# A block end's last sums: rounding the upper channels ahead of the quotient, and summing them between two steps of a numerator

## The chip, the cores and the metric

One core of one Trainium2 chip. The metric is the device time of one execution in microseconds (us), median of several runs; one more execution is profiled.

## What is computed

A causal convolution over the sequence (7 taps per head, softmaxed weights), then two dense layers of 192 -> 2048 -> 192 over 8192 tokens, each with a gate on the hidden value:

```python
x = attn_out.reshape(B * S, D)                  # B*S = 8192, D = 192
h = x @ w_in                                    # first layer, w_in 192 x 2048
x = (h * np.clip(h + 3.0, 0.0, 6.0) / 6.0) @ w_out
h = x @ w_in2                                   # second layer
P = a[0] + a[1]*h + a[2]*h**2 + a[3]*h**3       # numerator
Q = 1.0 + abs(b[0])*abs(h) + abs(b[1])*h**2     # denominator
out = (P / (Q + 1e-06)) @ w_out2
```

## The kernel before

Tokens are worked in 16 blocks of 512 (`BLK`), the hidden dimension in 16 tiles of 128 (`NF`), so there are 256 tiles per layer. The 192 channels are split into 128 lower ones ("a") and 64 upper ones ("b"). Each fp32 value is split into a rounded high part (fp32r) and the rest, a low part, and the products are made of several fp32r passes: in_product (L315) has five matmuls of 512 columns per tile, out_product (L327, 328, 329 into `ya_acc`, L332, 333 into `yb_acc`) five more. The two halves (partitions 0 to 63 and 64 to 127) of `yb_acc` are both sums for the same 64 upper channels, and must be added at the end of a block.

The two layers run interleaved. `run` walks a course of steps; step p works tile p of layer 1 and tile s = p - 20 of layer 2, and in each step every engine issues, in the order of its own list in a plan (`START`, `BEGIN`, `RAMP`, `MIDDLE`, `TURN`, `END`), what is due. `MIDDLE` holds from p = 30 to p = 257; from 258 `TURN` or `END`. In a list, ("num1", 1) is the tile s - 1 of layer 2; ("x2b_hi", SUM1, 0) is a step once per block k, issued in the first step with p - SUM1 - 0 >= 16 k, SUM1 being 18. No engine ever leaves its order; whoever waits holds up what stands behind it.

TensorE in a step of `MIDDLE`: in1(p), in2(s), out1(p-2), out2(s-4), 20 matmuls. The layer-1 hidden values have one PSUM bank only (`kept`), so in1(p+1) waits for gate1(p), which reads it (L402). in2 has three banks.

ScalarE per step: rsq2 (L456), relu1 (L395), rec2 (L468, writes the square of rsq, a first guess of 1/Q, over the h bank, and so waits for num1, the last reader of h), sq2 (L435), abs2 (L429), lin2 (L423), g1hi and g2hi (L507: round the gated values of layers 1 and 2; g2hi(s-2) waits for out2(s-4), the last reader of its buffer).

VectorE per step: num2 (L441), num1 (L446), the second and third steps of the numerator's Horner scheme; g_neg (L486, finishes the quotient), gate1 (L402), newton (L472), g_first (L479); in some steps one to three convolution taps (L599, L612) and cs_b_lo (L513). The taps of the upper channels are worked for two blocks at a time, all ahead of blocks of even number.

GpSimd per step: den_sum (L452), g1lo (L416), g2lo (L501), the low parts.

Once per block, in the step whose out1(p-2) is the first tile of the next block (p = 18 + 16 k), the sums of layer 1 leave PSUM: y1a_out (ScalarE, L521), x2a_hi (ScalarE, L507), x2a_lo (GpSimd, L515) for the lower channels; x2b_hi (ScalarE, L507: rounds `yb_acc[0][0:64]` into `xb_hl[1]`; the profile's y0b_acc and x1b_hl), x2b_res (VectorE, L542: what the rounding left, into partitions 64 to 127 of `x2b_rest`) and x2b_lo (VectorE, L547: adds the other half of `yb_acc`) for the upper ones. In that same step the first out1 of the new block may only start on `ya_acc` after y1a_out, and on `yb_acc` (its fourth matmul, L332) after x2b_lo. Both x2b_hi and y1a_out need the last out1 of the block, which TensorE ran one step earlier.

Of the kernel before, what the change touches and what calls it, by code (L numbers as in the profile page):

```python
# [34 lines left out]
SUM1, SUM2 = 16 + OUT1, 20  # L35
AHEAD, PAIR_AHEAD = -16, -32
# [32 lines left out]
MIDDLE = {  # L69
    "sync": [("load_a", AHEAD, 0), ("load_b", PAIR_AHEAD, 0, 0), ("store_y", SUM2, 1)],  # L70
    "tensor": [("in1", 0), ("in2", 0), ("out1", 2), ("out2", 4)],
    "scalar": [("y2b_move", SUM2, 0), ("y2a_out", SUM2, 0), ("x2b_hi", SUM1, 0), ("cs_b_hi", AHEAD, 13, 0),
             ("conv_a_first", AHEAD, -1), ("y1a_out", SUM1, 0), ("rsq2", 1), ("relu1", 0), ("x2a_hi", SUM1, 0),
             ("rec2", 1), ("conv_b_first", PAIR_AHEAD, 11, 0), ("sq2", 0), ("abs2", 0),
             ("cs_b_hi", AHEAD, 5, 1), ("lin2", 0), ("cs_a_hi", AHEAD, 10), ("g1hi", 0), ("g2hi", 2)],
    "vector": [("num2", 1), ("num1", 1), ("cs_b_lo", AHEAD, 15, 0), ("x2b_res", SUM1, 0),
             ("x2b_lo", SUM1, 0), ("y2b_sum", SUM2, 0), ("g_neg", 2), ("gate1", 0), ("newton", 1),
             ("cs_b_lo", AHEAD, 10, 1), ("conv_a", AHEAD, (1, 4, 5, 6, 7, 8)),
             ("conv_b_head", PAIR_AHEAD, (11, 13, 14), 0), ("conv_b_tail", AHEAD, (10, 11, 12), 0),
             ("g_first", 1)],  # L80
# [874 lines left out]
```

## Time and profile before

| | |
|---|---|
| median of 3 runs | 1211.4 us (1211.37 to 1211.76) |
| profiled execution | 1210.91 us, its span 1209.1 us |
| busy: TensorE / weight loads | 98% / 79% |
| busy: VectorE / ScalarE / GpSimd | 96% / 97% / 89% |
| granted TensorE clock, mean | 0.999 |

The span runs from the first to the last instruction. A matmul in the records lasts 0.39 us, but the next starts 0.23 us after it: they overlap, so a busy share of 98% does not say that the array streams without holes; the holes are seen in start times. Weight loads overlap the matmul before them. The granted clock is at its higher level, 2.4 GHz, throughout.

### The profile page before, as it was taken

What the parts mean: (1) busy time and instruction counts of PE and PEld (TensorE: products, weight loads), DVE (VectorE), ACT (ScalarE), POOL (GpSimd) and SP (SyncE); (2) the same over time, 40 slices, a digit from 0 to 9 for tenths busy, and PEclk for the clock granted to TensorE, in tenths of its full rate; (3) what the DMA queues carried; (4) which work ended last, traced back from release to release, by engine and by line L of the source; (5) the groups of instructions that cost most, each with busy time, mean ns of one, the idle gap of its engine ahead of it and who ended that gap; (6) DMA issues with size and microseconds to landing.
All of it is one profiled execution on the core that took longest, in us unless ns stands there. A gap on an engine that the chain in (4) does not pass through costs nothing.

```text
span 1209.1 us, 18307 instructions
## 1 busy us (share of the span) xinstructions
PE 1179.0 (98%) x5136; PEld 961.1 (79%) x5136; DVE 1158.8 (96%) x1786; ACT 1171.2 (97%) x2233; POOL 1070.8 (89%) x832
## 2 busy tenths in 40 slices
PE   6999999999999999999999999999999999999976
PEld 5778788888888888888888888888888888888754
DVE  7899999999999999999999999999999999999898
ACT  7899999999999999999999999999999999999997
POOL 5879989899998999989898998989989899998876
PEclk9999999999999999999999999999999999999999
DMA  4400000000000000010000000000000000000000
GB/s 147 150 1 10 1 23 1 23 10 23 1 1 26 6 23 1 1 32 1 23 1 21 11 1 23 1 23 10 1 23 1 23 1 14 1 1 14 1 14 14
DMA packets 10021, 21.17 MB, mean 18 GB/s; under 512 B 1600, under 2 KB 1856, under 8 KB 9920
## 3 DMA queue, kind: packets, MB, share of 16 engines
q1 hardware_dynamic: 9632, 20.00, 5.7%
q8 instruction: 40, 0.66, 0.2%
q14 instruction: 61, 0.50, 0.1%
q10 hardware_dynamic: 288, 0.01, 0.0%
HBM read 13.72 MB, written 6.29 MB: 17 GB/s over the span
## 4 chain that ended last, share of the span: by engine, by line
PE 78%; ACT 9%; DVE 6%; issue 5%; POOL 2%; DMA 0%; ACTq 0%; POOLq 0%; DVEq 0%
PE h L315 39%; PE y0b_acc L332 4%; PE y0b_acc L333 4%; PE y0a_acc L327 4%; PE y0a_acc L329 4%; PE y0a_acc L328 4%; PE y1a_acc L327 4%; PE y1a_acc L328 4%; PE y1a_acc L329 4%; PE y1b_acc L332 4%; PE y1b_acc L333 4%; ACT g_hi L507 2%; ACT num L423 1%; ACT sqr L435 1%; DVE num L441 1%
## 5 line engine op out<-in xcount | busy, mean ns | idle before, releaser
L452 POOL TENSOR_TENSOR den<-den,sqr 128x512 f32<-128x512 f32 x246 | 355.5, 1445 | 96.8 <-ACT den L429 92.6
L501 POOL TENSOR_TENSOR g_lo<-g,g_hi 128x512 fp32r<-128x512 f32 x255 | 331.0, 1298 | 2.5 <-ACT g_hi L507 2.5
L416 POOL TENSOR_TENSOR g_lo<-r,g_hi 128x512 fp32r<-128x512 f32 x235 | 308.7, 1314 | 4.5 <-ACT g_hi L507 2.8
L446 DVE SCALAR_TENSOR_TENSOR num<-num,coef,h 128x512 f32<-128x512 f32 x246 | 183.9, 748 | 8.4
L479 DVE SCALAR_TENSOR_TENSOR h<-num,coef,h 128x512 f32<-128x512 f32 x238 | 178.1, 748 | 0.2
L441 DVE TENSOR_TENSOR num<-num,h 128x512 f32<-128x512 f32 x246 | 167.9, 683 | 10.3 <-ACT num L423 4.4
L507 ACT ACTIVATE g_hi<-g 128x512 fp32r<-128x512 f32 x256 | 167.0, 652 | 10.2 <-DVE g L486 2.4
L423 ACT ACTIVATE num<-h,coef 128x512 f32<-128x512 f32 x246 | 175.0, 711 | 0.2
L402 DVE SCALAR_TENSOR_TENSOR r<-r,h 128x512 f32<-128x512 f32 x235 | 160.8, 684 | 9.2 <-ACT r L395 8.4
L456 ACT ACTIVATE rsq<-den 128x512 f32<-128x512 f32 x246 | 157.5, 640 | 7.8 <-POOL den L452 5.2
L486 DVE SCALAR_TENSOR_TENSOR g<-den,h 128x512 f32<-128x512 f32 x238 | 161.8, 680 | 0.7
L472 DVE SCALAR_TENSOR_TENSOR den<-den,h 128x512 f32<-128x512 f32 x238 | 161.8, 680 | 0.7 <-ACT h L468 0.4
L507 ACT ACTIVATE g_hi<-r 128x512 fp32r<-128x512 f32 x235 | 155.3, 661 | 0.0
L395 ACT ACTIVATE r<-h 128x512 f32<-128x512 f32 x256 | 153.8, 601 | 1.4 <-PE h L315 1.4
L435 ACT ACTIVATE sqr<-h 128x512 f32<-128x512 f32 x246 | 149.5, 608 | 1.4
L429 ACT ACTIVATE den<-h 128x512 f32<-128x512 f32 x246 | 150.3, 611 | 0.0
L468 ACT ACTIVATE h<-rsq 128x512 f32<-128x512 f32 x240 | 146.6, 611 | 0.8 <-DVE conv_b L446 0.2
L327 PE MATMUL y1a_acc<-g_hi,wout 128*128 128x512 f32 x255 | 100.8, 395 | 10.3 <-POOL g_lo L501 7.8
L315 PE MATMUL h<-x1a_hi,win_hi 128*128 128x512 f32 x256 | 100.1, 391 | 2.7 <-DVE g L486 2.4
L332 PE MATMUL y0b_acc<-g_hi,wout 128*128 128x512 f32 x256 | 101.0, 395 | 1.7 <-DVE x1b_hl L547 1.2
L327 PE MATMUL y0a_acc<-g_hi,wout 128*128 128x512 f32 x256 | 100.1, 391 | 2.4 <-DVE g_lo L416 1.4
L315 PE MATMUL h<-x0a_hi,win_hi 128*128 128x512 f32 x256 | 100.8, 394 | 0.7 <-DVE y1b_acc L402 0.4
(143 smaller groups left out, 2970.9 us busy)
## 6 DMA issues: line engine op xcount, KB each, us to landing
stage_w<-w_pack SPq DMA_DIRECT2D x16, 448.0 KB, 3.4
raw_a<-x_a SPq DMA_DIRECT2D x16, 259.0 KB, 3.2
out<-y_a SPq DMA_DIRECT2D x16, 256.0 KB, 2.0
out<-y_b SPq DMA_DIRECT2D x16, 128.0 KB, 2.3
raw_b<-x_b SPq DMA_DIRECT2D x14, 129.5 KB, 2.7
raw_b<-x_b SPq DMA_DIRECT2D x4, 65.5 KB, 4.7
tap_ab<-taps ACTq DMA_DIRECT2D x1, 7.0 KB, 3.3
coef<-coefs ACTq DMA_DIRECT2D x1, 3.0 KB, 4.2
```

What stands on the lines that cost most here:

```text
L315: mm = eng.matmul(psum, w, x[:, :], start=(i == 0), stop=(i == len(passes) - 1))
L327: eng.matmul(ya_acc[l][:, :], a_hi, g_hi[:, :], start=first, stop=False)
L332: eng.matmul(yb_acc[l][:, :], b_hl, g_hi[:, :], start=first, stop=False)
L416: eng.tensor_tensor(g1_lo[t % 2][:, :], gated(t)[:, :], f32(g1_hi[t % 2][:, :]), ALU.subtract).then_inc(S["g1lo"], 1)
L423: eng.activation(num_of(t), h2_of(t), ACT.Identity, bias=a2, scale=reg_a3) \
L441: eng.tensor_tensor(n, n, h2_of(t), ALU.mult).then_inc(S["num2"], 1)
L446: eng.scalar_tensor_tensor(out=n, in0=n, scalar=a1, in1=h2_of(t), op0=ALU.add, op1=ALU.mult).then_inc(S["num1"], 1)
L452: eng.tensor_tensor(den_of(t), den_of(t), sqr_of(t), ALU.add).then_inc(S["den_sum"], 1)
L472: eng.scalar_tensor_tensor(out=den_of(t), in0=den_of(t), scalar=Q_ONE, in1=quotient(t), op0=ALU.add, op1=ALU.mult).then_inc(S["newton"], 1)
L479: eng.scalar_tensor_tensor(out=quotient(t), in0=num_of(t), scalar=a0, in1=quotient(t), op0=ALU.add, op1=ALU.mult).then_inc(S["g_first"], 1)
L501: eng.tensor_tensor(g2_lo[t % 2][:, :], g2[t % 2][:, :], f32(g2_hi[t % 2][:, :]), ALU.subtract).then_inc(S["g2lo"], 1)
L507: return eng.activation(dst, src, ACT.Copy)
```

## The change

Two lists of the steady plan `MIDDLE` are edited. On ScalarE x2b_hi leaves its place near the head of the list (step p = 18 + 16 k, between y2a_out and cs_b_hi, ahead of y1a_out) and is issued one step earlier, at the end of step 17 + 16 k, between g1hi and g2hi. On VectorE x2b_res and x2b_lo move from behind num1 (and cs_b_lo) to between num2 and num1, in the same step as before. Nothing is added or left out; the other plans stand as they were.

```diff
 MIDDLE = {
-    "scalar": [("y2b_move", SUM2, 0), ("y2a_out", SUM2, 0), ("x2b_hi", SUM1, 0), ("cs_b_hi", AHEAD, 13, 0),
+    "scalar": [("y2b_move", SUM2, 0), ("y2a_out", SUM2, 0), ("cs_b_hi", AHEAD, 13, 0),
...
-             ("cs_b_hi", AHEAD, 5, 1), ("lin2", 0), ("cs_a_hi", AHEAD, 10), ("g1hi", 0), ("g2hi", 2)],
-    "vector": [("num2", 1), ("num1", 1), ("cs_b_lo", AHEAD, 15, 0), ("x2b_res", SUM1, 0),
-             ("x2b_lo", SUM1, 0), ("y2b_sum", SUM2, 0), ("g_neg", 2), ("gate1", 0), ("newton", 1),
+             ("cs_b_hi", AHEAD, 5, 1), ("lin2", 0), ("cs_a_hi", AHEAD, 10), ("g1hi", 0),
+             ("x2b_hi", SUM1, -1), ("g2hi", 2)],
+    "vector": [("num2", 1), ("x2b_res", SUM1, 0), ("x2b_lo", SUM1, 0), ("num1", 1),
+             ("cs_b_lo", AHEAD, 15, 0), ("y2b_sum", SUM2, 0), ("g_neg", 2), ("gate1", 0), ("newton", 1),
```

## Rows read from the trace of the kernel before

**Rows 1.** The page's part 4: the chain that ended last, by engine and line.
```profile
PE 78%; ACT 9%; DVE 6%; issue 5%; POOL 2%; DMA 0%; ACTq 0%; POOLq 0%; DVEq 0%
```

**Rows 2.** Waits of weight loads, 130 to 1136 us: us in total, times, longest.
```profile
PEld y0b_acc L332 <- DVE x1b_hl L547: 4.6, 13, 0.5
```

**Rows 3.** Timeline of matmuls (start, duration, us): first of two steps, block 6's end.
```profile
486.37 0.39 PE L315 MATMUL h<-x0a_hi,win_hi 128*128 128x512 f32 x1
...
491.29 0.39 PE L315 MATMUL h<-x0a_hi,win_hi 128*128 128x512 f32 x1
```

**Rows 4.** Timeline of weight loads there, [idle before <- releaser]: y0b_acc's, in1's of next step.
```profile
489.57 0.19 PEld L332 LDWEIGHTS y0b_acc<-g_hi,wout 128*128 128x128 f32 x1 [0.51 <-DVE x1b_hl L547]
...
491.06 0.19 PEld L315 LDWEIGHTS h<-x0a_hi,win_hi 128*128 128x128 f32 x1
```

**Rows 5.** Timeline of VectorE there: num2, num1, x2b_res, x2b_lo, g_neg, gate1; num1, g_neg.
```profile
486.61 0.68 DVE L441 TENSOR_TENSOR num<-num,h 128x512 f32<-128x512 f32 x1
487.32 0.75 DVE L446 SCALAR_TENSOR_TENSOR num<-num,coef,h 128x512 f32<-128x512 f32 x1
488.10 0.68 DVE L542 TENSOR_TENSOR x2b_rest<-y0b_acc,x1b_hl 64x512 f32<-64x512 f32 x1
488.82 0.69 DVE L547 TENSOR_TENSOR x1b_hl<-x2b_rest,y0b_acc 64x512 fp32r<-64x512 f32 x1
489.55 0.69 DVE L486 SCALAR_TENSOR_TENSOR g<-den,h 128x512 f32<-128x512 f32 x1
490.15 0.68 DVE L402 SCALAR_TENSOR_TENSOR r<-r,h 128x512 f32<-128x512 f32 x1
...
492.72 0.75 DVE L446 SCALAR_TENSOR_TENSOR num<-num,coef,h 128x512 f32<-128x512 f32 x1
493.38 0.68 DVE L486 SCALAR_TENSOR_TENSOR g<-den,h 128x512 f32<-128x512 f32 x1
```

**Rows 6.** Timeline of ScalarE there: g1hi, g2hi, x2b_hi, y1a_out; rec2.
```profile
485.94 0.71 ACT L507 ACTIVATE g_hi<-r 128x512 fp32r<-128x512 f32 x1
486.63 0.63 ACT L507 ACTIVATE g_hi<-g 128x512 fp32r<-128x512 f32 x1
487.17 0.57 ACT L507 ACTIVATE x1b_hl<-y0b_acc 64x512 fp32r<-64x512 f32 x1
487.65 0.58 ACT L521 ACTIVATE y_a<-y0a_acc 128x512 f32<-128x512 f32 x1
...
489.64 0.59 ACT L468 ACTIVATE h<-rsq 128x512 f32<-128x512 f32 x1
```

**Rows 7.** Timeline of all engines at block 7's end, from g1hi to in1's next step.
```profile
558.76 0.64 ACT L507 ACTIVATE g_hi<-r 128x512 fp32r<-128x512 f32 x1
...
559.24 0.68 DVE L441 TENSOR_TENSOR num<-num,h 128x512 f32<-128x512 f32 x1
...
559.29 0.39 PE L315 MATMUL h<-x0a_hi,win_hi 128*128 128x512 f32 x1
...
559.55 0.63 ACT L507 ACTIVATE g_hi<-g 128x512 fp32r<-128x512 f32 x1 [0.15 <-PE y1b_acc L333]
...
562.20 0.19 PEld L332 LDWEIGHTS y0b_acc<-g_hi,wout 128*128 128x128 f32 x1 [0.23 <-DVE x1b_hl L547]
...
563.93 0.39 PE L315 MATMUL h<-x0a_hi,win_hi 128*128 128x512 f32 x1
```

**Rows 8.** Timeline at block 1's end: y0b_acc's weights, gate1, in1's weights.
```profile
125.54 0.19 PEld L332 LDWEIGHTS y0b_acc<-g_hi,wout 128*128 128x128 f32 x1 [0.84 <-DVE x1b_hl L547]
...
126.12 0.68 DVE L402 SCALAR_TENSOR_TENSOR r<-r,h 128x512 f32<-128x512 f32 x1
...
127.03 0.19 PEld L315 LDWEIGHTS h<-x0a_hi,win_hi 128*128 128x128 f32 x1
```

**Rows 9.** Timeline at block 15's end: x2a_hi on ScalarE, the weights behind x2a_lo.
```profile
1143.63 0.63 ACT L507 ACTIVATE x1a_hi<-y_a 128x512 fp32r<-128x512 f32 x1
...
1145.68 0.19 PEld L315 LDWEIGHTS h<-x1a_lo,win_hi 128*128 128x128 f32 x1 [1.00 <-POOL x1a_lo L515]
```

## The prediction

> **What bounds the kernel now.** I read the chain of work that ended last first: TensorE holds 78% of it, ScalarE 9% and VectorE 6% [rows 1], so a change of order on ScalarE and VectorE pays only where TensorE waits for them. Then the waits of TensorE's weight loads in the steady stretch, 130 to 1136 us. It shows that one edge repeats there: 13 times, once for each block end in it, the weights of the first matmul into y0b_acc wait for x2b_lo (the L547 instruction on VectorE), 4.6 us in all [rows 2]. Those are the places the change touches.
>
> 4.6 us isn't yet the loss. One step of the plan is 20 matmuls; in the undisturbed ones they follow each other every 0.227 us, 4.53 us a step. An ordinary weight load has 0.04 us of idle before it (0.227 less its 0.19). The step at the end of block 6 takes 491.29 - 486.37 = 4.92 us [rows 3], 0.39 too long, while its weight load shows 0.51 idle [rows 4]; the step at the end of block 7 takes 563.93 - 559.29 = 4.64, 0.11 too long, with 0.23 idle [rows 7]. In both the loss is the idle time less 0.12: of a late release, 0.08 us beyond the usual 0.04 is free. 4.6 - 13 x 0.12 = 3.0 us is then what TensorE really loses in this stretch. By kind: six block ends like block 6 (even blocks, where num2 comes 0.24 into the step and not 0.05 ahead of it [rows 3, 5, 7], VectorE having the convolution of a pair of blocks behind it) at 0.39 = 2.3, six like block 7 at 0.11 = 0.65, and the last, at 1074 us, under 0.1: 3.0 again. Block 1, ahead of that stretch, has 0.84 us idle [rows 8], 0.72 lost by the same rule (I take 0.70). So all that can be won at this wait is about 3.7 us, 0.3% of the time.
>
> **What moves, at an even block's end (block 6).** Four facts from [rows 5]: num2 to num1, which depends on it, is 0.71 from start to start; num1 to x2b_res 0.78 and x2b_lo to g_neg 0.73, neither of which depends on the one before, so VectorE doesn't overlap these; x2b_res to x2b_lo 0.72. Elsewhere num1 to g_neg is 0.66 (492.72 to 493.38) and g_neg to gate1 0.60: there the next one starts before the last has ended. From num2 to g_neg the present order takes 489.55 - 486.61 = 2.94.
>
> ScalarE first. g2hi starts 0.69 after g1hi, where 0.54 separates two such steps (486.63 to 487.17) [rows 6]; in block 7 the same hole is marked 0.15, a wait for TensorE's out2 [rows 7]. x2b_hi, needing only the block's last out1, which ran five matmuls before out2's end, goes into that hole: 485.94 + 0.54 = 486.48, finished 0.57 later at 487.05. g2hi follows at 486.96 instead of 486.63, its reader on GpSimd being still busy with g1lo until after 488.4, and y1a_out starts at 487.50 instead of 487.65. No instruction is added or taken; ScalarE gains the 0.15.
>
> VectorE: num2 still at 486.61. x2b_res, like x2b_lo and what follows x2b_lo, I price without overlap (0.71, 0.72, 0.73), since their neighbours of the present order go that way: 487.32, by when x2b_hi has been done for 0.27; x2b_lo 488.04, ended 488.73 instead of 489.51; num1 488.77, g_neg 489.43, gate1 490.03 instead of 490.15. VectorE gains 0.12 only. The other end for this price is 0.60 for each of the outer two, the overlapped row, which would gain 0.36.
>
> Here a rule bears that could speak against the change. The Trainium skill, VectorE: DVE Perf Modes, section "Two Vector instructions with no wait between them", says in my words that an instruction is held until all earlier ones have finished when its first input or its output starts in another quadrant of 32 partitions than the last one in the same memory. x2b_res writes partition 64, x2b_lo reads it, num1 goes back to 0: three held instructions in the new order as in the old. The trace agrees with it at 0.78 and 0.73 against 0.66 and 0.60 [rows 5]. By the rule VectorE gains 0.12 a block and the sum is the one below; without it VectorE gains 0.36, even blocks give 0.39 and block 1 0.6, and the sum would be 3.5, 1207.9.
>
> Now TensorE. Its y0b_acc weights would be wanted at 489.57 less 0.47, 489.10 [rows 4]; x2b_lo is ready at 488.73 plus 0.06 (release to start, 489.51 to 489.57). The 0.39 goes, with 0.3 to spare. What is late next: in1 of the next step, which has a single h bank and waits for gate1. Its weights come at 491.06 now and at 490.67 then [rows 4]; gate1 ends at 490.03 + 0.68 = 490.71, released 490.77. That is 0.10 late, of which 0.08 is free: 0.02 lost. So an even block gives 0.37, and six of them **2.2 us**. This is a near thing: 0.1 us more on VectorE comes back to TensorE whole.
>
> The displaced num1: ScalarE's rec2 waits for it, and sq2, abs2 and the rest are queued behind rec2. num1 ends at 489.52, rec2 would otherwise start at 489.64 - 0.15 = 489.49 [rows 6]; it starts at 489.58. That eats 0.09 of ScalarE's gain. newton, the reader, comes behind gate1 at 490.63 anyway. ScalarE and VectorE are then 0.3 us later against TensorE than before; in an ordinary step ScalarE has eight instructions at 0.54 or less from start to start [rows 6], under 4.3 us of TensorE's 4.53, so that closes in a step or two.
>
> **Odd blocks (block 7).** g1hi 558.76, x2b_hi 559.30 to 559.88; num2 559.24, x2b_res 559.95, x2b_lo 560.67 to 561.36 instead of 562.14; gate1 ends 563.34. in1's weights come a matmul ahead of it, 563.93 - 0.23 = 563.70 now and 563.59 then: nothing late [rows 7]. Six times 0.11, **0.65 us**, and the end at 1074 us 0.07.
>
> **Block 1.** 0.70 goes; an earlier wait of TensorE for y1a_out in the same step stays, as ScalarE has no hole there and y1a_out keeps its place. gate1 is at 126.12 less 0.12, ends at 126.68, released 126.74; in1's weights would come at 127.03 - 0.70 = 126.33 [rows 8]. 0.41 late, 0.33 lost. Net **0.37 us**; ends 0 and 0.70.
>
> **Block 15**, at the turn to the last stage. The step count reaches x2b_hi one step earlier than that stage's own list, so the steady list places it: ahead of g2hi and y1a_out instead of behind them. x2a_hi, now at 1143.63 [rows 9], has y1a_out straight before it: that starts 0.48 later (one slot, 487.17 to 487.65 [rows 6]), at 1143.15, lasts its 0.58, and x2a_hi starts 0.06 behind its end, at 1143.79, 0.16 later; g2lo delays x1a_lo on GpSimd a little more, and TensorE waits there for it [rows 9], but the waits that follow hang on ScalarE's chain. Cost **0.16 us**; ends 0 and 0.48.
>
> Sum: 2.2 + 0.65 + 0.07 + 0.37 - 0.16 = 3.1 us. Profiled execution 1210.91 (span 1209.1, 1.8 around it) becomes 1207.8; the median of the runs stands 0.5 above it, so 1211.4 - 3.1 = **1208.3**.
>
> **Rivals.** (1) Given back to gate1. What VectorE's new order takes longer than worked out comes out of the even blocks one for one: 0.12 if it gains nothing. For it: the margin is 0.02 us. Against it: each duration has a row. Price: with gate1 0.25 later than worked out, even blocks and block 1 give 0.12 each, and 7 x 0.12 + 0.72 - 0.16 = 1.4: 1210.0. (2) Slower: x2b_hi doesn't come earlier to VectorE. If ScalarE reaches it as late as now (1.38 into the step), x2b_res waits, with num1, g_neg and gate1 queued behind, work that fills this time today. In odd blocks x2b_res stays at 559.24 + 0.71 + 0.78 = 560.73; x2b_lo 561.45, num1 562.18, g_neg 562.84, gate1 563.44 to 564.12, released 564.18 against 563.70: 0.48 less 0.08 is lost beyond today's 0.11. The same walk in even blocks gives 0.11 + 0.41 instead of 0.39, and 0.4 at the last: 6 x 0.4 + 6 x 0.13 + 0.4 + 0.16 = 3.8 us, 1215.2. It decides once x2b_hi ends some 0.4 us later than 559.88. Against it: g1hi is done before TensorE's release at both kinds of block end [rows 6, 7]. (3) More: block 1 whole, the turn free, and even blocks at 0.39: 0.70 + 2.34 + 0.72 = 3.8, and a little of the y1a_out wait with it: 4.0, 1207.4. (4) It does nothing, because another wait ends at the same moment as x2b_lo: in block 6 y1a_out ends at 487.65 + 0.58 = 488.23 [rows 6], 0.87 before those weights are wanted, so I hold this unlikely; 1211.4.
>
> **How the numbers follow.** The forecast, 1207.6 to 1209.0, 0.60; rival 1 with all between 1209.0 and 1211, 0.22; slower, 0.08; more, 0.05; nothing, 0.05. About 0.2%, 2.4 us, is what can be told from no change: faster 0.65 (the forecast and rival 3), same 0.27, slower 0.08. Range 1207.3 to 1210.9, which holds the forecast, rival 3 and nearly all of rival 1.
>
> **What would show it.** Right: the weight loads wait for x2b_lo (L547) nowhere between 130 and 1136 us; block 6's step is 4.55 and block 7's 4.53; x2b_res follows num2 by 0.71 and num1 follows x2b_lo by 0.73; no new edge from in1 (L315) to r (L402) over 0.15, but at block 1; x1a_lo at the turn 0.2 to 0.3 later. Wrong: such an edge in all even blocks (rival 1); x2b_rest waiting for ScalarE for over 0.3 us in odd blocks (rival 2); a new wait of TensorE three to fourteen steps behind a block end, which would mean that ScalarE doesn't catch up.

## The result

| | median of 9 runs | range |
|---|---|---|
| before | 1211.4 us | 1211.01 to 1211.86 |
| after | 1208.24 us | 1207.74 to 1208.36 |

The ratio is 0.9973, with a 95% interval of 0.9963 to 0.9983: 3.2 us. The median is clear of the 0.2% that the prediction took for the least that can be told from no change; the weak end of the interval, 0.17% or 2.1 us, lies just under it. 1208.3 was predicted.

The page of the kernel after, part 4, the chain that ended last:

```profile
PE 91%; ACT 4%; issue 2%; DVE 1%; DMA 0%; POOL 0%; POOLq 0%; ACTq 0%; DVEq 0%
```

Against 78, 9 and 6% in [rows 1]: ScalarE and VectorE have nearly left the chain. The view that answers to [rows 2], who held up the weight loads between 130 and 1136 us, and the same edge in the kernel before:

```profile
PEld h L316 <- DVE r L403: 0.9, 3, 0.4
```

```profile
PEld h L315 <- DVE r L402: 0.7, 2, 0.4
```

The 13 waits for x2b_lo are gone (in the changed file every line behind the lists stands one lower, L548 for L547). What is left is three waits of in1 for gate1, L403, the edge that the prediction named as next. Two of them, at 1036.5 and 1041.2 us, lie away from the block ends and stood in the kernel before as well. One is new, at block 2's end:

```profile
199.72 0.19 PEld L316 LDWEIGHTS h<-x0a_hi,win_hi 128*128 128x128 f32 x1 [0.20 <-DVE r L403]
```

At the other even block ends in1's weights are up to 0.1 us late, too little for this view.

Block 6's end, timelines of matmuls, weight loads, VectorE and ScalarE after, which answer to [rows 3] to [rows 6]:

```profile
485.49 0.39 PE L316 MATMUL h<-x0a_hi,win_hi 128*128 128x512 f32 x1
...
490.02 0.40 PE L316 MATMUL h<-x0a_hi,win_hi 128*128 128x512 f32 x1
...
494.57 0.39 PE L316 MATMUL h<-x0a_hi,win_hi 128*128 128x512 f32 x1
```

```profile
489.57 0.19 PEld L334 LDWEIGHTS y1b_acc<-g_lo,wout 128*128 128x128 f32 x1
489.89 0.19 PEld L316 LDWEIGHTS h<-x0a_hi,win_hi 128*128 128x128 f32 x1
```

```profile
485.74 0.68 DVE L442 TENSOR_TENSOR num<-num,h 128x512 f32<-128x512 f32 x1
486.45 0.69 DVE L543 TENSOR_TENSOR x2b_rest<-y0b_acc,x1b_hl 64x512 f32<-64x512 f32 x1
487.17 0.69 DVE L548 TENSOR_TENSOR x1b_hl<-x2b_rest,y0b_acc 64x512 fp32r<-64x512 f32 x1
487.89 0.75 DVE L447 SCALAR_TENSOR_TENSOR num<-num,coef,h 128x512 f32<-128x512 f32 x1
488.56 0.68 DVE L487 SCALAR_TENSOR_TENSOR g<-den,h 128x512 f32<-128x512 f32 x1
489.15 0.68 DVE L403 SCALAR_TENSOR_TENSOR r<-r,h 128x512 f32<-128x512 f32 x1
```

```profile
485.06 0.71 ACT L508 ACTIVATE g_hi<-r 128x512 fp32r<-128x512 f32 x1
485.58 0.62 ACT L508 ACTIVATE x1b_hl<-y0b_acc 64x512 fp32r<-64x512 f32 x1
486.06 0.66 ACT L508 ACTIVATE g_hi<-g 128x512 fp32r<-128x512 f32 x1
486.58 0.62 ACT L522 ACTIVATE y_a<-y0a_acc 128x512 f32<-128x512 f32 x1
...
488.74 0.60 ACT L469 ACTIVATE h<-rsq 128x512 f32<-128x512 f32 x1
```

The step lasts 490.02 - 485.49 = 4.53 instead of 4.92 and the next 4.55. x2b_res follows num2 by 0.71, x2b_lo 0.72 later, num1 0.72, g_neg 0.67, gate1 0.59. gate1 ends at 489.15 + 0.68 = 489.83 and in1's weights start at 489.89; at the ordinary spacing behind the load at 489.57 they would have come at 489.80. They are 0.09 late, and 0.02 is lost in the next step: the prediction said 0.10 and 0.02. g1hi, x2b_hi, g2hi and y1a_out follow each other at 0.52, 0.48, 0.52; the hole is filled. rec2 is 3.25 into the step, against 3.27 before. It is held by num1, which ends at 488.64.

Where the time went, from starts of in1 in the two traces:

| stretch | before | after | difference | predicted |
|---|---|---|---|---|
| block 1's end, steps 34 and 35 | 10.15 | 9.71 | -0.44 | -0.37 |
| from step 36 to the matmul at 1133.05 us, 11 us ahead of the turn's first wait | 1001.25 | 998.43 | -2.82 | -2.9 |
| from there to the last matmul | 71.57 | 71.75 | +0.18 | +0.16 |

Together this is 3.08 us. The span of the profiled execution fell by 2.6 only, because in it step 34 came 0.41 later (122.07 against 121.66 us). That is start-up, which the change doesn't touch: it varied between 121.4 and 123.2 us in the profiles of this study.

### The profile page after: what moved, and what is told of

Same layout as the page of the kernel before. It is cut to its first block, busy times and chain, and to the rows that moved or that the text cites. A ratio compares the mean times of both kernels' runs of the same rounds, so it can differ in the third digit from the quotient of the medians.

```text
span 1206.5 us, 18307 instructions
## 1 busy us (share of the span) xinstructions
PE 1176.7 (98%) x5136; PEld 961.7 (80%) x5136; DVE 1156.9 (96%) x1786; ACT 1170.5 (97%) x2233; POOL 1074.8 (89%) x832
## 4 chain that ended last, share of the span: by engine, by line
PE 91%; ACT 4%; issue 2%; DVE 1%; DMA 0%; POOL 0%; POOLq 0%; ACTq 0%; DVEq 0%
PE h L316 45%; PE y0a_acc L328 5%; PE y0a_acc L329 5%; PE y0b_acc L334 5%; PE y0b_acc L333 5%; PE y0a_acc L330 5%; PE y1a_acc L328 4%; PE y1b_acc L334 4%; PE y1a_acc L329 4%; PE y1b_acc L333 4%; PE y1a_acc L330 4%; ACT g_hi L508 1%; ACT num L424 1%; ACT sqr L436 0%; DMA coef<-coefs 0%
## 5 line engine op out<-in xcount | busy, mean ns | idle before, releaser
L453 POOL TENSOR_TENSOR den<-den,sqr 128x512 f32<-128x512 f32 x246 | 359.6, 1462 | 92.2 <-ACT den L430 88.0
L403 DVE SCALAR_TENSOR_TENSOR r<-r,h 128x512 f32<-128x512 f32 x235 | 161.0, 685 | 8.2 <-ACT r L396 6.3
```

The lines of the kernel that those rows point to most:

```text
L453: eng.tensor_tensor(den_of(t), den_of(t), sqr_of(t), ALU.add).then_inc(S["den_sum"], 1)
```

## Experiments

Each changes the kernel after unless something else is said. "Two steps" is the time from in1 at the block end to in1 two steps later; twice 20 matmuls at 0.2267 us are 9.07. Before, this was 9.45 at block 6 and 9.16 at block 5; after, 9.09 and 9.07.

### One half of the change at a time

ScalarE's half alone:

```diff
-    "vector": [("num2", 1), ("x2b_res", SUM1, 0), ("x2b_lo", SUM1, 0), ("num1", 1),
-             ("cs_b_lo", AHEAD, 15, 0), ("y2b_sum", SUM2, 0), ("g_neg", 2), ("gate1", 0), ("newton", 1),
+    "vector": [("num2", 1), ("num1", 1), ("cs_b_lo", AHEAD, 15, 0), ("x2b_res", SUM1, 0),
+             ("x2b_lo", SUM1, 0), ("y2b_sum", SUM2, 0), ("g_neg", 2), ("gate1", 0), ("newton", 1),
```

> ScalarE's half of the change alone: x2b_hi between g1hi and g2hi, VectorE in the order of before. Theory (the time goes at x2b_lo, and x2b_lo is late because num1 stands ahead of it on VectorE): x2b_res starts 0.78 after num1 in the trace of before although x2b_hi has been done for 0.36 us in even blocks, so x2b_lo stays where it was; even steps 4.92 us, odd 4.64, the last block end (where x2b_res did wait for ScalarE) gains 0.07, the turn costs 0.16: 1211.5 us. Rival (the early rounding is what pays, VectorE's order is an extra): half of the 3.2 us or more, under 1210 us, with even steps under 4.75.

1211.06 us beside 1211.03 for the kernel before on the same chip, ratio 1.0001 (0.9991 to 1.0010). ScalarE, then VectorE at block 6's end:

```profile
488.13 0.61 ACT L508 ACTIVATE x1b_hl<-y0b_acc 64x512 fp32r<-64x512 f32 x1
```

```profile
489.00 0.75 DVE L447 SCALAR_TENSOR_TENSOR num<-num,coef,h 128x512 f32<-128x512 f32 x1
489.77 0.69 DVE L543 TENSOR_TENSOR x2b_rest<-y0b_acc,x1b_hl 64x512 f32<-64x512 f32 x1
```

x2b_hi is done at 488.74, a full 1.03 us before x2b_res, which stands behind num1 and starts 0.77 after it as ever. Steps at even block ends take 4.96 to 4.97 us, 0.04 more than expected, and at odd ones 4.62 to 4.64. Only at the last block end, where x2b_res did wait for ScalarE, do two steps fall from 9.15 to 9.07, as expected. An early rounding alone is worth nothing; the rival falls.

VectorE's half alone, made from the kernel before:

```diff
-    "vector": [("num2", 1), ("num1", 1), ("cs_b_lo", AHEAD, 15, 0), ("x2b_res", SUM1, 0),
-             ("x2b_lo", SUM1, 0), ("y2b_sum", SUM2, 0), ("g_neg", 2), ("gate1", 0), ("newton", 1),
+    "vector": [("num2", 1), ("x2b_res", SUM1, 0), ("x2b_lo", SUM1, 0), ("num1", 1),
+             ("cs_b_lo", AHEAD, 15, 0), ("y2b_sum", SUM2, 0), ("g_neg", 2), ("gate1", 0), ("newton", 1),
```

> VectorE's half alone: x2b_res and x2b_lo between num2 and num1, x2b_hi behind g2hi as before. Theory: slower than before. x2b_res waits for x2b_hi with num1, g_neg and gate1 queued behind it, and in1 of the next step waits for gate1: odd steps 4.64 + 0.40 = 5.04 us, even steps 4.53 + 0.11 + 0.41 = 5.05, the last block end 0.4 more; with 6 x 0.40 + 6 x 0.13 + 0.4 that is 3.6 us over before, 1215.0 us, and x2b_rest is seen to wait for ScalarE 0.6 to 0.7 us in odd blocks. Rival (x2b_lo ahead of num1 is all that counts): 0.3 to 0.6 us of x2b_lo's lateness goes and the time falls by 1 to 3 us, 1208.4 to 1210.4.

1213.91 us, ratio 1.0024 (1.0014 to 1.0034): 2.9 us slower than before. VectorE at block 5's end, and the waits of 130 to 1136 us:

```profile
414.41 0.68 DVE L441 TENSOR_TENSOR num<-num,h 128x512 f32<-128x512 f32 x1
415.87 0.69 DVE L542 TENSOR_TENSOR x2b_rest<-y0b_acc,x1b_hl 64x512 f32<-64x512 f32 x1 [0.78 <-ACT x1b_hl L507]
416.58 0.69 DVE L547 TENSOR_TENSOR x1b_hl<-x2b_rest,y0b_acc 64x512 fp32r<-64x512 f32 x1
```

```profile
DVE x2b_rest L542 <- ACT x1b_hl L507: 8.2, 13, 1.1
PEld h L315 <- DVE r L402: 7.6, 15, 0.5
...
PEld y0b_acc L332 <- DVE x1b_hl L547: 2.5, 13, 0.2
```

This is the prediction's slower rival, made real. x2b_lo's lateness does fall, from 4.6 to 2.5, but VectorE stands 8.2 us idle with num1, g_neg and gate1 behind it (0.78 us at odd blocks, 0.39 or a little more at even ones), and TensorE meets gate1 late at all 13 block ends; with the two old waits this is 7.6. The size was 2.9 and not 3.6: two steps take 9.51 to 9.56 at either kind of block end, mostly 0.45 too long, where 0.51 and 0.52 were expected (x2b_res starts 0.03 behind x2b_hi's end, not 0.07), and block 1 gained 0.09. The direction and the mechanism hold. So neither half gives anything, one costs 2.9, and both together win 3.2. The halves don't add: each takes away what the other would wait for.

### How near the next edge is

A memset of 64 x 160 (and in a second kernel 64 x 32) between x2b_lo and num1, once per block:

```diff
+        def pad(eng, k):
+            eng.memset(x2b_rest[0:DB, 0:160], 0.0)
...
-    "vector": [("num2", 1), ("x2b_res", SUM1, 0), ("x2b_lo", SUM1, 0), ("num1", 1),
+    "vector": [("num2", 1), ("x2b_res", SUM1, 0), ("x2b_lo", SUM1, 0), ("pad", SUM1, 0), ("num1", 1),
...
```

> The changed kernel with one added VectorE instruction of duration d per block, a memset of 64x160 between x2b_lo and num1, nothing else. Theory (gate1 is the next to be late, with 0.02 us over in even blocks and 0.27 in odd ones, counting the 0.08 us of lateness that is free): even steps grow by d + 0.03 - 0.06, odd steps not at all while d + 0.03 is under 0.27; at d = 0.25 this is 6 x 0.22, and 0.28 at block 1: 1.6 us, 1209.8 us. Rival (VectorE has real room behind a block end, the even blocks' step of 4.53 is no edge): under 0.4 us in all, 1208.3 to 1208.6.

> As e5_pad_160 with 32 columns instead of 160. There the memset took 0.19 us, num1 came 0.29 later in even blocks, and an even step and its next lost 0.28 together. Theory (the edge lies where the changed kernel stands, one for one from there on): about 0.13 less delay, 0.16 in even blocks, lost whole, 6 x 0.15 + 0.16 at block 1 = 1.1 us over the changed kernel, 1209.0; odd blocks nothing. Rival (0.08 us of lateness is free, as assumed in the prediction): 6 x 0.08 + 0.16 = 0.6 us.

64 x 160: 1210.16 beside 1211.03, ratio 0.9993 (0.9983 to 1.0002). 64 x 32: 1209.19 beside 1211.29, ratio 0.9982 (0.9973 to 0.9991). So 2.3 and 1.1 us of the 3.2 are lost. VectorE at block 6's end in the first, then in the second:

```profile
487.72 0.69 DVE L548 TENSOR_TENSOR x1b_hl<-x2b_rest,y0b_acc 64x512 fp32r<-64x512 f32 x1
488.50 0.19 DVE L553 MEMSET x2b_rest<- 64x160 f32 x1
488.70 0.75 DVE L447 SCALAR_TENSOR_TENSOR num<-num,coef,h 128x512 f32<-128x512 f32 x1
```

```profile
487.53 0.69 DVE L548 TENSOR_TENSOR x1b_hl<-x2b_rest,y0b_acc 64x512 fp32r<-64x512 f32 x1
488.29 0.09 DVE L553 MEMSET x2b_rest<- 64x32 f32 x1
488.38 0.75 DVE L447 SCALAR_TENSOR_TENSOR num<-num,coef,h 128x512 f32<-128x512 f32 x1
```

num1 stands 0.98 and 0.85 behind x2b_lo instead of 0.72. Two steps at block 6 take 9.36 and 9.23 instead of 9.09: 0.27 lost for 0.26 of added distance, 0.14 for 0.13. At block 5 they take 9.08 and 9.07 instead of 9.07. That is one for one in even blocks and next to nothing in odd ones. The 1.6 us expected of the longer pad came out at 2.3. The free 0.08 us is used up already where the kernel after stands (0.09 late, 0.02 lost), and the expectation had taken 0.06 off each even block for it all the same; block 1 adds 0.33, and odd blocks 0.01 to 0.03 each. The 1.1 of the shorter one, expected with that corrected, came out at 1.1, and its rival, 0.6, falls. In even blocks the gain of this change is as large, to 0.02 us, as VectorE lets it be in this order.

Where the lateness goes, from the weights and the first matmul of the next step with the shorter pad:

```profile
490.38 0.19 PEld L316 LDWEIGHTS h<-x0a_hi,win_hi 128*128 128x128 f32 x1 [0.29 <-DVE r L403]
```

```profile
490.38 0.50 PE L316 MATMUL h<-x0a_hi,win_hi 128*128 128x512 f32 x1
```

The weights are 0.29 - 0.04 = 0.25 late and the two steps 9.23 - 9.07 = 0.16 too long, so 0.08 or 0.09 is still free. The matmul starts with its weights and is on record for 0.50 us instead of 0.39: that is why most of the loss shows only in the step behind.

### What an instruction on the upper partitions costs

x2b_res writes partitions 64 to 127. Let it write 0 to 63:

```diff
-            eng.tensor_tensor(x2b_rest[DB:P, :], yb_acc[0][0:DB, :], f32(xb_hl[1][k % 2][0:DB, :]),
+            eng.tensor_tensor(x2b_rest[0:DB, :], yb_acc[0][0:DB, :], f32(xb_hl[1][k % 2][0:DB, :]),
...
-            eng.tensor_tensor(xb_hl[1][k % 2][DB:P, :], x2b_rest[DB:P, :], yb_acc[0][DB:P, :],
+            eng.tensor_tensor(xb_hl[1][k % 2][DB:P, :], x2b_rest[0:DB, :], yb_acc[0][DB:P, :],
```

> The changed kernel with x2b_rest in partitions 0 to 63 instead of 64 to 127, so that x2b_res writes where the instructions ahead of it write. Theory (x2b_res doesn't overlap num2 because its output starts at another quadrant): num2 to x2b_res 0.60 instead of 0.71 us in even blocks, x2b_res to x2b_lo 0.72 and x2b_lo to num1 0.73 as they are; gate1 0.11 earlier in even blocks, 0.02 in odd ones, where x2b_res then waits for x2b_hi; 0.1 to 0.2 us of time, 1208.1 us. Rival (64 rows, or the wait on ScalarE's semaphore, is what stops the overlap): 0.71 as before and no time.

```profile
485.39 0.68 DVE L442 TENSOR_TENSOR num<-num,h 128x512 f32<-128x512 f32 x1
485.99 0.67 DVE L543 TENSOR_TENSOR x2b_rest<-y0b_acc,x1b_hl 64x512 f32<-64x512 f32 x1
486.70 0.69 DVE L548 TENSOR_TENSOR x1b_hl<-x2b_rest,y0b_acc 64x512 fp32r<-64x512 f32 x1
```

0.60 instead of 0.71 from num2 to x2b_res, with 64 rows as before and the same semaphore: neither is what stopped the overlap, the output's first partition is. 1207.69 us beside 1211.03, 3.3 under before. The kernel after is 3.2 under it, and 0.15 us between two such figures is less than they can tell; but two steps at block 6 are 9.07, so the last 0.02 is gone.

Then the other edge, x2b_lo to num1. All halves are exchanged, so that x2b_lo writes the lower partitions and num1 could overlap it:

```diff
-            round_hi(eng, xb_hl[1][k % 2][0:DB, :], yb_acc[0][0:DB, :]).then_inc(S["x2b_hi"], 1)
+            round_hi(eng, xb_hl[1][k % 2][DB:P, :], yb_acc[0][DB:P, :]).then_inc(S["x2b_hi"], 1)
...
-            eng.tensor_tensor(x2b_rest[DB:P, :], yb_acc[0][0:DB, :], f32(xb_hl[1][k % 2][0:DB, :]),
+            eng.tensor_tensor(x2b_rest[0:DB, :], yb_acc[0][DB:P, :], f32(xb_hl[1][k % 2][DB:P, :]),
...
-            eng.tensor_tensor(xb_hl[1][k % 2][DB:P, :], x2b_rest[DB:P, :], yb_acc[0][DB:P, :],
+            eng.tensor_tensor(xb_hl[1][k % 2][0:DB, :], x2b_rest[0:DB, :], yb_acc[0][0:DB, :],
```

> The changed kernel again, on the chip of the three that follow, as their measure. Both theories: 3.1 us under before, as measured first.

> The changed kernel with the halves exchanged: the rounded part goes to partitions 64 to 127 (from y0b_acc's upper half), the rest to 0 to 63 of x2b_rest, and x2b_lo writes partitions 0 to 63 from inputs in 0 to 63, where num1's operands lie. Theory (what stops the overlap is a change of the start quadrant of the first input or of the output, and not the 64 rows): now x2b_res is held (0.71 us behind num2, as in the changed kernel) and num1 is free, 0.60 behind x2b_lo instead of 0.73. g_neg, gate1 and rec2 come 0.12 earlier in every block, odd ones too. TensorE: the rest of the even blocks' loss and 0.12 at block 1 and half of the 0.1 in block 2: 0.2 us under the changed kernel, hardly more than its measurement can tell. Rival (a 64-row instruction is never overlapped with its next): num1 at 0.73, no difference.

The kernel after again: 1207.84 beside 1211.03, 3.2 under it. The exchange: 1211.15, ratio 1.0002 (0.9993 to 1.0011). All of the gain is gone. VectorE at block 5's end does what was expected:

```profile
415.16 0.68 DVE L548 TENSOR_TENSOR x1b_hl<-x2b_rest,y0b_acc 64x512 fp32r<-64x512 f32 x1
415.77 0.73 DVE L447 SCALAR_TENSOR_TENSOR num<-num,coef,h 128x512 f32<-128x512 f32 x1
```

num1 follows x2b_lo by 0.61 instead of 0.72. But ScalarE, at block 6's end, and the weight loads there:

```profile
486.08 0.72 ACT L508 ACTIVATE g_hi<-r 128x512 fp32r<-128x512 f32 x1
486.82 0.59 ACT L508 ACTIVATE x1b_hl<-y0b_acc 64x512 fp32r<-64x512 f32 x1
487.44 0.63 ACT L508 ACTIVATE g_hi<-g 128x512 fp32r<-128x512 f32 x1
488.10 0.60 ACT L522 ACTIVATE y_a<-y0a_acc 128x512 f32<-128x512 f32 x1
```

```profile
488.81 0.19 PEld L328 LDWEIGHTS y0a_acc<-g_hi,wout 128*128 128x128 f32 x1 [0.57 <-POOL g_lo L417]
```

0.74, 0.62 and 0.66 from start to start, where the kernel after has 0.52, 0.48 and 0.52: moved to the upper partitions, x2b_hi doesn't overlap the one ahead of it, g2hi doesn't overlap x2b_hi, nor y1a_out g2hi. That is half a microsecond more, and y1a_out ends at 488.70, after the weights of y0a_acc were due at 488.28 (488.81 less 0.53). The label names GpSimd's g_lo, which ended at 488.60; this load waits for y1a_out too, which ended later, 0.11 ahead of it. The stall has moved from y0b_acc to y0a_acc: two steps take 9.49. Odd blocks keep their gain (9.10 at block 5), but the stretch from the matmul ahead of the turn to the last one is 72.21 us instead of 71.75. I expected a gain because I had asked which instructions VectorE overlaps, and not whether the same holds for ScalarE. The trace of before had a case of it: y2b_move (the y_b line), which reads the upper half, is not overlapped on either side.

```profile
514.22 0.63 ACT L507 ACTIVATE g_hi<-g 128x512 fp32r<-128x512 f32 x1 [0.15 <-PE y1b_acc L333]
514.88 0.60 ACT L562 ACTIVATE y_b<-y1b_acc 64x512 f32<-64x512 f32 x1
515.50 0.60 ACT L554 ACTIVATE y_a<-y1a_acc 128x512 f32<-128x512 f32 x1
```

### The turn

The steady list passes over x2b_hi in its last step, p = 257, so that the turn's own list places it, as before the change:

```diff
                 for stage, lag, *at in plan[name]:
+                    if stage == "x2b_hi" and p == END_AT - 1:
+                        continue
```

> The changed kernel, but block 15's x2b_hi stays in the turn's own list, behind y1a_out, as before. Theory: x2a_hi comes right behind its place of before, x1a_hi's and x1a_lo's weights at the turn are 0.1 to 0.2 us earlier than in the changed kernel against the step's start, and 0.1 to 0.2 us of time is won. Rival (the waits behind the turn hang on another chain and swallow it): nothing beyond the turn's first two waits, the same time as the changed kernel within 0.05.

1207.69 beside 1211.03, 3.3 under it. The first two waits at the turn, in the kernel after, then in this one:

```profile
1141.68 0.19 PEld L316 LDWEIGHTS h<-x1a_hi,win_hi 128*128 128x128 f32 x1 [0.85 <-issue]
1143.07 0.19 PEld L316 LDWEIGHTS h<-x1a_lo,win_hi 128*128 128x128 f32 x1 [1.10 <-POOL x1a_lo L516]
```

```profile
1140.96 0.19 PEld L316 LDWEIGHTS h<-x1a_hi,win_hi 128*128 128x128 f32 x1 [0.70 <-issue]
1142.26 0.19 PEld L316 LDWEIGHTS h<-x1a_lo,win_hi 128*128 128x128 f32 x1 [1.00 <-POOL x1a_lo L516]
```

0.15 and 0.10 less idle, and 71.57 us from the matmul ahead of the turn to the last one, as before the change, instead of 71.75. The rival (swallowed later) falls: the 0.18 is real, though the time alone couldn't show it.

> Both of the last two together, as a version that should beat the changed kernel: by theory 0.2 + 0.15 us under it, 3.5 us under before. Rival: one or none of the two, under 0.2.

1211.00 beside 1211.03, 0.15 under the exchange alone, where 3.5 under before was expected: the exchange had taken it all. The turn's part is there again in the trace, 72.03 us instead of 72.21 from the matmul ahead of the turn to the last one.

> The changed kernel with x2b_rest in partitions 0 to 63 and with block 15's x2b_hi left in the turn's own list. Theory: 0.16 us by the first (in e3_rest_low the stretch from in1 of step 35 to the turn was 0.16 shorter) and 0.18 by the second (in e8_turn_kept the stretch behind the turn was as long as before): 3.4 to 3.5 us under before, the best of all. Rival (the two hang on the same wait): 0.2 under the changed kernel at most.

1207.67 beside 1211.29, ratio 0.9969 (0.9957 to 0.9981): 3.6 us under before, the largest difference of the study (3.4 to 3.5 was expected). Two steps at block 6 are 9.07 and the stretch behind the turn is 71.57. It isn't shown to beat the kernel after by time (0.4 us apart in different comparisons, whose intervals overlap); by its trace it has both small losses removed.

## Why the prediction was right

- **The bound.** "13 times at one edge, 3.0 us really lost" held: from block 3 on two steps at a block end are down to 9.07 to 9.10, and 2.8 us of it are measured between step 36 and the turn. The reading that mattered was not to take the 4.6 us of the wait for the loss.
- **Even blocks**, 0.37 predicted: 9.454 - 9.087 = 0.367. Its parts held too: VectorE's three unoverlapped neighbours (0.71, 0.72, 0.72) and gate1 0.09 late. The pads show that the margin was read rightly; priced with overlap, the step would have promised an ease that wasn't there.
- **Odd blocks**, 0.11 predicted: 9.160 - 9.067 = 0.09 at block 5. **Block 1**: 0.44 against 0.37. Its leftover reaches block 2: from step 41 to step 50 num2 stays 0.08 to 0.09 later against TensorE than before (0.32 into step 50, 0.23 before), in1's weights are late there and 0.09 is lost. This is most of what 2.82 lacks to 2.9, and it is the one new edge over 0.15 away from block 1, which the prediction had ruled out. That block 1 gave 0.07 too much and block 2 0.09 too little is why the sum came out nearer than its parts, which is luck.
- **num1 and rec2**: the wait exists (rec2 at 3.25, not at 3.12 into the step) and costs nothing on TensorE.
- **Catching up** was misjudged. ScalarE and VectorE were to be level again against TensorE in a step or two behind an even block; they need five and six. Step 118, four behind block 6's end, in1 and num2, before and after:

```profile
504.89 0.39 PE L315 MATMUL h<-x0a_hi,win_hi 128*128 128x512 f32 x1
504.99 0.68 DVE L441 TENSOR_TENSOR num<-num,h 128x512 f32<-128x512 f32 x1
```

```profile
503.64 0.39 PE L316 MATMUL h<-x0a_hi,win_hi 128*128 128x512 f32 x1
504.13 0.68 DVE L442 TENSOR_TENSOR num<-num,h 128x512 f32<-128x512 f32 x1
```

  num2 is 0.10 into the step before and 0.49 after, and level only in step 121 (1.17 in both). rec2 on ScalarE is 0.26 to 0.38 later until step 119. No wait of TensorE comes of it, so the sum is untouched; what sets the pace of the two engines there stays open.
- **The turn**: 0.18 against 0.16, and undone by e8_turn_kept. The path held too: x2a_hi starts 0.14 later against TensorE, where 0.16 was predicted, and the weights behind x2a_lo come 0.23 later, where 0.2 to 0.3 was.
- **The slower rival** was a real one, and only ScalarE's half of the change keeps it away. The prediction priced it at 3.8, with the turn's 0.16 in it; VectorE's half alone cost 2.9.

The range held the time, and its upper part (gate1 giving back up to 2 us) was no idle caution: 0.13 us per block on VectorE cost 1.1 us in e4_pad_32.

## What to carry to other kernels

When a bound engine waits for a result at the end of two engines' queues, follow it back through both orders: moving the consumer ahead of unrelated work pays only if its producer moves too, and moving one of them can cost nearly as much as both win, 2.9 us against 3.2 here. Cost a stall by the length of the period around it, not by the idle time in the waits view, and look up what is released next, with its margin, before adding the gains. Before an operand is moved to other partitions, look at what that does to the spacing on every engine that touches it.

## What the runs showed of the hardware

ScalarE overlaps successive instructions only in part of the cases: 0.48 to 0.52 us from start to start for 512 columns, but 0.62 to 0.74 before and behind an instruction whose input and output lie in partitions 64 to 127, among others that start at 0 (e6_swap, at every block end), and 0.62 to 0.66 around one that only reads from there (y2b_move). The 64 rows are not the reason: the same x2b_hi in partitions 0 to 63 is overlapped, 0.48 to 0.52. On VectorE it is 0.60 against 0.71 to 0.73, and moving the output of one instruction from partition 64 to 0 was enough to change it. For VectorE the Trainium skill has this as a rule (VectorE: DVE Perf Modes, section "Two Vector instructions with no wait between them"): what counts is the quadrant of 32 partitions in which inputs and output start. It takes every input and not only the first, as the prediction has it; here this makes no difference, since the inputs of x2b_res, of x2b_lo and of num1 each start in one quadrant. Both of its cases that were tried agree, x2b_res at 0.60 in e3_rest_low and num1 at 0.61 in e6_swap. Which of input and output does it on ScalarE was not taken apart.

In these runs a weight load that started up to 0.1 us after its turn cost TensorE 0.03 us at most, and a later one its lateness less 0.07 to 0.09: at block 6's end 0.02 us was lost when it was 0.09 late, 0.16 when 0.25 late (e4_pad_32) and 0.29 when 0.38 late (e5_pad_160), part of it in the step behind.
